# A delta-rule attention and two expert layers on one core: units of three chunks of two sequences, wider scan steps, no filler products in the first unit

## The chip, the cores and the metric

The kernel runs on one core of a Trainium2 chip. The metric is the device time of one execution in microseconds (us); lower is better. The engines named below are TensorE (PE in the rows; its weight loads are PEld), VectorE (DVE), ScalarE (ACT), GpSimd (POOL) and SyncE (SP, which here only issues DMAs).

## What is computed

All data are fp32. The first part is a recurrence along each of 4 x 8 sequences of 768 positions with heads of 48; it is computed in chunks of 64 positions. The second part is a gated dense layer on 3072 tokens of 384 values with 1536 hidden columns. The third sends each token with a positive skip score to one of 8 experts.

```python
# attention: for every batch and head, t = 0 .. 767
y[t] = q[t] @ state
v_old = state.T @ kn[t]                     # kn: k divided by its norm
state += beta[t] * outer(kn[t], v[t] - v_old)
# dense layer: x is y, laid out as 3072 tokens x 384
x = (sigmoid(x @ w_gate) * (x @ w_val)) @ w_out
# experts: rows with x @ w_skip > 0 go to e = argmax(x @ w_gate2)
out = x;  out[row] = x[row] + softmax_weight * (relu(x[row] @ w1[e]) @ w2[e])
```

## The kernel before

The work is cut into Q = 8 units of CT = 384 tokens. A unit of the kernel before is JU = 6 chunks of 64 positions of one batch entry, all 8 heads; two units in a row make a sequence. For each unit TensorE makes the scores of keys and queries (stage `gram`, L682), VectorE masks them (`pt`, L468, and `mask`, L475 to L482), turns them to lanes (L485) and solves the triangular system of every chunk in 30 dependent steps of two instructions (`solve`, L489 and L491). `from_lanes` (L493 to L496) turns the result back; `off` (L698, L712) and `wu` (L728, L731) are products that need it. Then comes the scan over the chunks, in which the state `st` passes from chunk to chunk: `read` (L746) multiplies the state, VectorE subtracts (L516), `write` (L763 and L771) multiplies again, VectorE adds to the state (L521) and ScalarE copies the outputs out (L619), and the next `read` waits for both. `x_turn` (L805 to L810) transposes the unit's outputs for the dense layer, whose pieces are `gate` (L824), `val` (L833) and `out` (L842), three products of 384 or 393 columns each; 12 gates, 12 vals and 12 outs make a unit's dense work.

Every engine runs its own instructions in order, and all of them walk through one list of stages that `program_order` writes. In that list the attention of unit q+1 lies between the dense pieces of unit q, so only unit 0's attention has nothing beside it. `dense(n)` appends pieces, `behind(n)` appends stages that only VectorE has (`lengths`, `mask`, `turn_in`, `solve`), each with a weight. A VectorE stage that stands ahead of another in the list also runs ahead of it, whatever TensorE does. In unit 0 the kernel before puts products that nobody reads (stage `warm`, L790: 128x256 by the identity) between the stages: 20 behind the `router` products (L782), 22 more from `off` to the last `write`, 42 in all.

A small product uses a part of the array (64x64 or 32x64), a dense one all of it. In TensorE's rows of the trace every fp32 product stands as two records, so x6 is three products. The experts' part (L993 to L1108) is not touched by the change.

## Time and profile before

| | us |
|---|---|
| median of 3 runs (lowest to highest) | 1058.85 (1058.5 to 1059.47) |
| the profiled execution | 1058.32 |
| its span in the profile | 1056.5 |
| TensorE busy | 990.5 (94%) |
| VectorE busy | 455.4 (43%) |
| ScalarE busy | 168.4 (16%) |
| GpSimd busy | 109.1 (10%) |

The span is the profiled part of one execution; 1.8 us of its time lie around it. Busy is the time in which an engine has an instruction in work. The first dense piece starts 88.47 us into the span, the last one ends about 834 us in, and the experts follow. TensorE is busy nearly all the time between those two points; ahead of the first it has long idle stretches.

### The profile page before, as it was taken

What the parts mean: (1) busy time and instruction counts of PE and PEld (TensorE: products, weight loads), DVE (VectorE), ACT (ScalarE), POOL (GpSimd) and SP (SyncE); (2) the same over time, 40 slices, a digit from 0 to 9 for tenths busy, and PEclk for the clock granted to TensorE, in tenths of its full rate; (3) what the DMA queues carried; (4) which work ended last, traced back from release to release, by engine and by line L of the source; (5) the groups of instructions that cost most, each with busy time, mean ns of one, the idle gap of its engine ahead of it and who ended that gap; (6) DMA issues with size and microseconds to landing.
All of it is one profiled execution on the core that took longest, in us unless ns stands there. A gap on an engine that the chain in (4) does not pass through costs nothing. (4 is left out here: it accounts for less than half of the span.)

```text
span 1056.5 us, 23056 instructions
## 1 busy us (share of the span) xinstructions
PE 990.5 (94%) x10065; PEld 661.8 (63%) x10065; DVE 455.4 (43%) x1130; ACT 168.4 (16%) x370; POOL 109.1 (10%) x137
## 2 busy tenths in 40 slices
PE   4899999999999999999999999999999539999997
PEld 3776655665665566556656655655555337878785
DVE  5958586385358427624843583112011111111121
ACT  2022211210221022112102210211110011111110
POOL 3010100101010110011010101000001112222221
PEclk9599999999999999999999999999999869999999
DMA  9502003000300210030003000000730104444410
GB/s 349 226 3 106 2 2 136 18 1 17 136 2 1 88 66 1 2 135 18 1 16 137 2 1 20 29 1 1 281 124 1 45 18 155 156 152 152 143 35 27
DMA packets 28859, 74.03 MB, mean 70 GB/s; under 512 B 3912, under 2 KB 19960, under 8 KB 27744
## 3 DMA queue, kind: packets, MB, share of 16 engines
q1 hardware_dynamic: 18672, 56.74, 14.6%
q10 hardware_dynamic: 6912, 9.55, 2.5%
q0 software_dynamic: 3184, 6.39, 2.0%
q8 instruction: 74, 1.21, 0.5%
q14 instruction: 17, 0.14, 0.0%
HBM read 60.62 MB, written 13.00 MB: 70 GB/s over the span
## 5 line engine op out<-in xcount | busy, mean ns | idle before, releaser
L842 PE MATMUL ps<-wo,prod 128*128 128x393 f32 x576 | 205.3, 503 | 3.6 <-DVE prod L535 3.2
L824 PE MATMUL ps<-xT,wg 128*128 128x384 f32 x576 | 205.9, 494 | 0.7 <-ACT xT L626 0.7
L833 PE MATMUL ps<-xT,wv 128*128 128x384 f32 x576 | 206.2, 494 | 0.0
L842 PEld LDWEIGHTS ps<-wo,prod 128*128 128x128 f32 x576 | 104.7, 189 | 74.6 <-DVE prod L535 6.5
L824 PEld LDWEIGHTS ps<-xT,wg 128*128 128x128 f32 x576 | 105.9, 190 | 68.7 <-issue 1.8
L833 PEld LDWEIGHTS ps<-xT,wv 128*128 128x128 f32 x576 | 105.6, 190 | 67.2 <-issue 1.0
L535 DVE TENSOR_TENSOR prod<-sig,ps 128x384 f32<-128x384 f32 x96 | 53.2, 554 | 213.5 <-PE ps L833 212.0
L1094 PEld LDWEIGHTS ps_h<-xgT,arena 128*128 128x128 f32 x816 | 95.0, 194 | 5.2 <-ACT xgT L1051 1.0
L1094 PE MATMUL ps_h<-xgT,arena 128*128 128x128 f32 x816 | 95.3, 277 | 0.6 <-ACT xgT L1051 0.6
L1106 PE MATMUL ps_y<-arena,hT 128*128 128x384 f32 x272 | 90.5, 486 | 0.0
L631 ACT ACTIVATE sig<-ps 128x384 f32<-128x384 f32 x96 | 47.1, 490 | 272.6 <-PE ps L824 272.6
L491 DVE TENSOR_TENSOR arena<-arena 128x30 f32<-128x30 f32 (+14 forms) x240 | 79.7, 332 | 8.2
L489 DVE TENSOR_TENSOR arena<-arena 128x30 f32<-128x30 f32 (+14 forms) x240 | 79.3, 330 | 6.6
L377 POOL DMA_INDIRECT lists<-token,slot x24 | 23.7, 986 | 481.9 <-DVE slot L568 477.1
L1106 PEld LDWEIGHTS ps_y<-arena,hT 128*128 128x128 f32 x272 | 50.4, 190 | 31.5
L349 POOL TENSOR_TENSOR length<-sq,half 128x24 f32<-128x24 f32 x8 | 33.4, 4181 | 296.7 <-DVE sq L452 296.7
L682 PE MATMUL ps<-arena 48*64 48x128 f32 x768 | 29.1, 308 | 17.9 <-DMA arena<-in_kq 9.0
L1041 DVE SCALAR_TENSOR_TENSOR yv<-ps_y,gate,xres 128x384 f32<-128x384 f32 x17 | 10.5, 618 | 81.8 <-PE ps_y L1106 81.8
L1030 DVE TENSOR_SCALAR hT<-ps_h 128x256 f32<-128x256 f32 x34 | 14.4, 425 | 65.7 <-PE ps_h L1094 65.7
L682 PEld LDWEIGHTS ps<-arena 48*64 48x64 f32 x768 | 25.7, 155 | 22.1 <-issue 18.5
L746 PEld LDWEIGHTS ps<-st,arena 48*64 48x64 f32 x1408 | 24.5, 134 | 23.2 <-issue 21.7
L728 PEld LDWEIGHTS ps<-tt,arena 64*64 64x64 f32 x768 | 33.5, 133 | 8.3 <-issue 4.9
(152 smaller groups left out, 835.3 us busy)
## 6 DMA issues: line engine op xcount, KB each, us to landing
arena<-in_moe_w SPq DMA_DIRECT2D x16, 1536.0 KB, 10.4
arena<-in_kq SPq DMA_DIRECT2D x8, 1536.0 KB, 7.6
x_scratch<-x ACTq DMA_DIRECT2D x24, 196.5 KB, 3.6
arena<-in_kr SPq DMA_DIRECT2D x8, 576.0 KB, 3.8
vr<-in_v SPq DMA_DIRECT2D x8, 576.0 KB, 10.0
out<-x ACTq DMA_DIRECT2D x24, 192.0 KB, 3.2
prod<-in_turned_moe_w_out SPq DMA_DIRECT2D x1, 2304.0 KB, 19.3
wo<-in_moe_w_out SPq DMA_DIRECT2D x1, 2304.0 KB, 25.0
```

Of the source, the lines that this page charges most:

```text
L349: nc.gpsimd.tensor_tensor(length[:], sq[:], half[:].to_broadcast([P, NS]), ALU.pow).then_inc(root_ready, 1)
L489: link(nc.vector.tensor_tensor(tv, xl[:, u + 1:H2, u:u + 1].to_broadcast([P, rows, u]), xl[:, u:u + 1, 0:u].to_broadcast([P, rows, u]), AL ...
L491: link(nc.vector.tensor_tensor(xl[:, u + 1:H2, 0:u], xl[:, u + 1:H2, 0:u], tv, ALU.add))
L535: nc.vector.tensor_tensor(prod[:, f, :], sig[:, f % 2, :], ps_m[3 - f % 2][:, 0:CT], ALU.mult)\
L631: nc.scalar.activation(sig[:, f % 2, :], ps_m[f % 2][:, 0:CT], ACT.Sigmoid).then_inc(sig_ready, 1)
L682: last = nc.tensor.matmul(banks[rows(h), c, n * 2 * C:(n + 1) * 2 * C], kq[part, q % 2, j, g, h, 0, :], kq[part, q % 2, j, g, h, :, :].rea ...
L728: nc.tensor.matmul(ps_a[rows(c), 2 + h, k * C:(k + 1) * C], kr[rows(h), q % 2, n * D:n * D + GP], tt[rows(h), n, :], start=True, stop=True)
L824: last = nc.tensor.matmul(ps_m[f % 2][:, 0:CT], wg[:, a, f * P:(f + 1) * P], xT[:, a, :], start=(a == 0), stop=(a == KT - 1))
L833: last = nc.tensor.matmul(ps_m[3 - f % 2][:, 0:CT], wv[:, a, f * P:(f + 1) * P], xT[:, a, :], start=(a == 0), stop=(a == KT - 1))
L842: last = nc.tensor.matmul(ps_m[t][:, 0:XW], prod[:, a, t * P:(t + 1) * P], wo[:, a, :], start=(a == 0), stop=(a == NF - 1))
L1094: last = nc.tensor.matmul(ps_h[f // 2][:, f % 2 * P:(f % 2 + 1) * P], w1[:, ws, a, f * P:(f + 1) * P], xgT[:, a, :], start=(a == 0), stop= ...
L1106: last = nc.tensor.matmul(ps_y[:, 0:DM], hT[:, f, :], w2[:, ws, f, :], start=(f == 0), stop=(f == FT - 1))
```

## The change

It regroups the work. A unit is now JS = 3 chunks of SEQ = 2 sequences (two batch entries), so the tokens of a unit, and the number of products, stay as they were, and four units in a row carry one pair of sequences. The scan has three steps per unit instead of six, each with twice the columns in every instruction: 32 products in a `read`, 16 and 16 in a `write`. The `warm` products are gone. In the list of stages: a dense piece now stands between `wu` and `gram`; VectorE's stages are paid out behind every dense piece in every region, at 0.8 per piece; the gap between scan steps is worked out from what dense work is left. In unit 0 the loads are cut and reordered (`load_first`), ScalarE copies the raw scores to SBUF (`raw`), VectorE's `pt` for units 0 and 1 moves behind the solve and behind the scan, and the first `mask` instruction no longer needs the scores. The output's rows are put back in order on the host. The diff, cut to its core:

```diff
-JU = 6
+JS = 3
+SEQ = 2
+JU = JS * SEQ
...
-    def dense(n):
-        owed[0] += n
-        while pieces and (owed[0] >= 0.5 or pieces[0][0] in light):
-            owed[0] -= pieces[0][0] not in light
-            order.append(pieces.pop(0))
     def behind(n):
         owed[1] += n
@@ -67,46 +64,47 @@
             event, w = later.pop(0)
             owed[1] -= w
             order.append(event)
+        owed[1] = min(owed[1], 0.0)
+    def dense(n):
+        owed[0] += n
+        while pieces and (owed[0] >= 0.5 or pieces[0][0] in light):
+            heavy = pieces[0][0] not in light
+            order.append(pieces.pop(0))
+            if heavy:
+                owed[0] -= 1
+                behind(0.8)
...
+        for j in range(JS):
+            s = q * JS + j
+            if s % (QS * JS):
+                steps.append(("read", s, j))
+            steps.append(("write", s, j))
...
-    order += [("norm", 0, 0), ("lengths", 0, 0), ("gram", 0, 0), ("gram", 0, 1), ("pt", 0, 0), ("gram", 0, 2), ("pt", 0, 1),
-              ("pt", 0, 2)] + [event for event, _ in prepare(0)[1:5]]
-    order += [("gram", 1, i) for i in range(3)] + [("router", 0, 0), ("warm", 0, 20)] + [event for event, _ in prepare(0)[5:]]
-    order += [("from_lanes", 0, 0), ("router_copy", 0, 0), ("off", 0, 0), ("pt", 1, 0), ("pt", 1, 1), ("warm", 1, 4),
-              ("off", 0, 1), ("norm", 1, 0), ("warm", 1, 3), ("wu", 0, 0), ("pt", 1, 2), ("warm", 1, 2), ("wu", 0, 1),
-              ("warm", 1, 2)]
+    order += [("norm", 0, 0)] + [("gram", 0, i) for i in range(3)] + [event for event, _ in prepare(0)[0:5]]
+    order += [("router", 0, 0)] + [("gram", 1, i) for i in range(3)]
+    order += [event for event, _ in prepare(0)[5:]]
+    order += [("from_lanes", 0, 0), ("router_copy", 0, 0), ("off", 0, 0), ("off", 0, 1)]
+    order += [("pt", 0, i) for i in range(3)] + [("wu", 0, 0), ("norm", 1, 0), ("wu", 0, 1)]
     later = prepare(1)
     for step in scan(0):
         order.append(step)
-        if step != scan(0)[-1]:
-            order.append(("warm", 1, 1))
-        behind(0.4)
-        owed[1] = 0.0
-    order += [("x_turn", 0, a) for a in range(KT)]
+        behind(0.5)
+    order += [("x_turn", 0, a) for a in range(KT)] + [("pt", 1, i) for i in range(3)]
...
-            lead = sum(w for _, w in later) / 0.82
             while later:
-                behind(0.82)
-                owed[1] = 0.0
                 dense(1.0)
             follows = q + 1 < Q
-            steps = scan(q)
-            gap = max(0.6, (32.0 - lead - 7.0) / len(steps))
...
             order.append(("wu", q, 1))
+            dense(1.0)
             if follows:
                 order += [("gram", q + 1, 0), ("gram", q + 1, 1), ("pt", q + 1, 0)]
                 dense(1.0)
                 order += [("gram", q + 1, 2), ("pt", q + 1, 1), ("pt", q + 1, 2)]
+                dense(0.7)
                 later = prepare(q + 1)
-            dense(0.7)
+            steps = scan(q)
+            gap = max(0.7, (sum(p[0] not in light for p in pieces) - 4.0) / len(steps))
             for step in steps:
                 order.append(step)
-                behind(0.86 * gap + 0.23)
                 dense(gap)
-                owed[1] = min(owed[1], 0.0)
...
-        first = 2 * (i + 1) if q == 1 else 2 * (i % 2)
+        first = 4 if (q, i) == (0, 2) else 2 * (i % 2)
...
+        load_first(0)
+        load_kr(0)
+        load_first(1)
+        load_first(2)
         sp.dma_start(bt[:], beta_d).then_inc(beta_in, 16)
-        load(0)
-        load(1)
+        sp.dma_start(wr[:, :, 0:1], ws_d.rearrange("(a p o) -> p a o", p=P, o=1), allow_slow_non_contiguous=True).then_inc(router_in, 16)
+        sp.dma_start(wr[:, :, 1:R1], wgt_d.rearrange("(a p) e -> p a e", p=P)).then_inc(router_in, 16)
+        sp.dma_start(wo_t, wo_t_d.rearrange("(a p) f -> p a f", p=P)).then_inc(router_in, 16)
+        load_kq(1)
+        load_kr(1)
         load_v(0)
-        sp.dma_start(wr[:, :, 0:1], ws_d.rearrange("(a p o) -> p a o", p=P, o=1), allow_slow_non_contiguous=True).then_inc(wo_in, 16)
-        sp.dma_start(wr[:, :, 1:R1], wgt_d.rearrange("(a p) e -> p a e", p=P)).then_inc(wo_in, 16)
-        sp.dma_start(wo_t, wo_t_d.rearrange("(a p) f -> p a f", p=P)).then_inc(wo_in, 16)
+        load_v(1)
         sp.dma_start(wo[:, :, 0:DM], wo_d.rearrange("(a p) f -> p a f", p=P)).then_inc(wo_in, 16)
-        load_v(1)
         sp.dma_start(wg[:], wg_d.rearrange("(a p) f -> p a f", p=P)).then_inc(w_in, 16)
...
-                dve.wait_ge(graw_copied, 3 * q + i + 1)
-                pair = gram_banks(q, i).rearrange("p c (j g a t) -> p c j g a t", j=2, g=G2, a=2)
-                own_pt = pt[:, q % 2].rearrange("p (c j g) t -> p c j g t", c=CG, g=G2)
+                own_pt = pt[:, q % 2].rearrange("p (c j g) t -> p c j g t", c=CG, g=G2)[:, :, 2 * i:2 * i + 2]
+                if q < 2:
+                    dve.wait_ge(raw_copied, 3 * q + i + 1)
+                    scores = own_pt
+                else:
+                    dve.wait_ge(graw_copied, 3 * q + i + 1)
+                    scores = gram_banks(q, i).rearrange("p c (j g a t) -> p c j g a t", j=2, g=G2, a=2)[:, :, :, :, 1, :]
                 nc.vector.tensor_tensor(
-                    own_pt[:, :, 2 * i:2 * i + 2], pair[:, :, :, :, 1, :],
-                    tri[:].unsqueeze(1).unsqueeze(1).to_broadcast([P, CG, 2, G2, C]), ALU.mult).then_inc(pt_ready, 1)
+                    own_pt, scores, tri[:].unsqueeze(1).unsqueeze(1).to_broadcast([P, CG, 2, G2, C]), ALU.mult)\
+                    .then_inc(pt_ready, 1)
...
                 diag = dg[:, 0:NS, :]
+                factors = dn[:, 0:NS, :]
                 if i == 0:
+                    if q:
+                        dve.wait_ge(y1_done, q)
+                    nc.vector.scalar_tensor_tensor(
+                        out=factors, in0=tri32[:].unsqueeze(1).to_broadcast([P, NS, H2]), scalar=-1.0,
+                        in1=bp[:, 0:NS].unsqueeze(2).to_broadcast([P, NS, H2]), op0=ALU.mult, op1=ALU.mult)
+                elif i == 1:
                     dve.wait_ge(upper_ready, q + 1)
                     link(nc.vector.scalar_tensor_tensor(out=diag, in0=graw[:, q % 2, :, H2:C], scalar=lower[:, 0:1], in1=diag,
                                                         op0=ALU.mult, op1=ALU.add))
-                elif i == 1:
-                    link(nc.vector.scalar_tensor_tensor(out=diag, in0=diag, scalar=-1.0,
-                                                        in1=bp[:, 0:NS].unsqueeze(2).to_broadcast([P, NS, H2]),
-                                                        op0=ALU.mult, op1=ALU.mult))
                 else:
-                    link(nc.vector.tensor_tensor(diag, diag, tri32[:].unsqueeze(1).to_broadcast([P, NS, H2]), ALU.mult))
+                    link(nc.vector.tensor_tensor(diag, diag, factors, ALU.mult))
...
+                u = u_of(s // JS, i)
+                nc.vector.tensor_tensor(u, u, ps_a[:, 0:2, 0:W4], ALU.subtract).then_inc(u_ready, 1)
             elif stage == "write" and (q + 1) % SB:
                 s = q
                 dve.wait_ge(s_done, writes(s))
                 if s % SB:
-                    nc.vector.tensor_tensor(st[:], st[:], ps_a[:, 2:4, 0:W2], ALU.add).then_inc(st_ready, 1)
+                    nc.vector.tensor_tensor(st[:], st[:], ps_a[:, 2:4, 0:W4], ALU.add).then_inc(st_ready, 1)
                 else:
-                    nc.vector.tensor_copy(st[:], ps_a[:, 2:4, 0:W2]).then_inc(st_ready, 1)
+                    nc.vector.tensor_copy(st[:], ps_a[:, 2:4, 0:W4]).then_inc(st_ready, 1)
...
+        def raw(q, i):
+            pair = gram_banks(q, i).rearrange("p c (n a t) -> p c n a t", n=2 * G2, a=2)
+            nc.scalar.activation(by_group(pt[:, q % 2], 2 * G2 * i, 2 * G2), pair[:, :, :, 1, :], ACT.Copy)\
+                .then_inc(raw_copied, 1)
...
+                if q == 1:
+                    raw(1, i)
+                elif q == 0 and i == 2:
+                    for third in range(3):
+                        raw(0, third)
...
+                if q == 0:
+                    pe.wait_ge(kq_first[i], 16)
+                elif i == 0:
+                    pe.wait_ge(kq_in[q % 2], 16 * ((q + 1) // 2))
+                if q >= 2 and i < 2:
+                    pe.wait_ge((u_evac, w_evac)[i], 2 * q)
+                elif q >= 2:
                     pe.wait_ge(pt_ready, 3 * q + 1)
+                elif q == 1:
+                    pe.wait_ge(raw_copied, (3, 3, 4)[i])
...
+                    for x in range(SEQ):
+                        for g in range(G2):
+                            for c in range(CG):
+                                part = slice(GP * c, GP * c + D)
+                                for h in range(HH):
+                                    o = x * W2 + g * D
+                                    last = nc.tensor.matmul(
+                                        ps_a[rows(h), c, a * W4 + o:a * W4 + o + D], kq[part, b, SEQ * i + x, g, h, a, :],
+                                        st[part, h, o:o + D], start=(a == 0 and x == 0 and g == 0), stop=(a == 0),
+                                        skip_group_check=True)
...
+                if s < JS and i == 0:
+                    pe.wait_ge(pt_ready, 3)
+                for x in range(SEQ):
                     for g in range(G2):
                         for c in range(CG):
-                            n = CN * c + G2 * i + g
+                            n, o = CN * c + G2 * (SEQ * i + x) + g, W4 + x * W2 + g * D
                             for h in range(HH):
-                                last = nc.tensor.matmul(ps_a[rows(c), 2 + h, g * D:(g + 1) * D],
-                                                        kr[rows(h), b, n * D:n * D + GP], vr[rows(h), b, n * D:(n + 1) * D],
-                                                        start=True, stop=True)
-                    last.then_inc(s_done, 1)
-                for g in range(G2):
-                    for c in range(CG):
-                        n = CN * c + G2 * i + g
-                        for h in range(HH):
-                            last = nc.tensor.matmul(ps_a[rows(h), c, W2 + g * D:W2 + (g + 1) * D], pt[rows(h), b, n, :],
-                                                    vr[rows(h), b, n * D:(n + 1) * D],
-                                                    start=(s % SB == 0 and g == 0), stop=True, skip_group_check=True)
+                                last = nc.tensor.matmul(
+                                    ps_a[rows(h), c, o:o + D], pt[rows(h), b, n, :], vr[rows(h), b, n * D:(n + 1) * D],
+                                    start=(s % SB == 0 and x == 0 and g == 0), stop=True, skip_group_check=True)
...
-            elif stage == "warm":
-                if q:
-                    pe.wait_ge(pt_ready, 5)
-                for _ in range(f):
-                    nc.tensor.matmul(ps_m[0][:, 0:2 * P] if q else ps_a[:, 1, 0:2 * P], ident[:], wo_t[:, 0, 0:2 * P],
-                                     start=True, stop=True)
```

TensorE's rows in the order of the program, first unit, from the `router` products on. Before, with L790 the products that nobody reads:

```order
L782 MATMUL ps<-wr,prod 128x9 x36
L790 MATMUL ps<-prod,ident 128x256 x20
L698 MATMUL ps<-arena 64x32 x48
L790 MATMUL ps<-prod,ident 128x256 x4
L712 MATMUL ps<-dt,y 64x32 x48
L790 MATMUL ps<-prod,ident 128x256 x3
```

The same place now, with L817 the router, L714 `gram`, L729 and L741 `off`:

```order
L714 MATMUL ps<-arena 64x128 x48
L817 MATMUL ps<-wr,prod 128x9 x36
L714 MATMUL ps<-arena 64x128 x48
L729 MATMUL ps<-arena 64x32 x48
L741 MATMUL ps<-dt,y 64x32 x48
```

The router moved ahead of unit 1's `gram`, and nothing stands between the stages.

TensorE's rows in the dense work of unit 0 from unit 2's `gram` on (L682), through the scan of unit 1 (L746 `read`, L763 and L771 `write`), before:

```order
L682 MATMUL ps<-arena 64x128 x16
L824 MATMUL ps<-xT,wg 128x384 x3
L746 MATMUL ps<-st,arena 64x48 x16
L833 MATMUL ps<-xT,wv 128x384 x3
L763 MATMUL ps<-vr,arena 64x48 x8
L771 MATMUL ps<-vr,arena 64x48 x8
L824 MATMUL ps<-xT,wg 128x384 x3
L746 MATMUL ps<-st,arena 64x48 x16
```

And now (L714 `gram`, L776 `read`, L795 and L806 `write`, L852, L861 and L872 the dense pieces):

```order
L861 MATMUL ps<-xT,wv 128x384 x3
L714 MATMUL ps<-arena 64x128 x32
L852 MATMUL ps<-xT,wg 128x384 x3
L714 MATMUL ps<-arena 64x128 x16
L861 MATMUL ps<-xT,wv 128x384 x3
L776 MATMUL ps<-st,arena 64x48 x32
L872 MATMUL ps<-wo,prod 128x393 x3
L795 MATMUL ps<-vr,arena 64x48 x16
L806 MATMUL ps<-vr,arena 64x48 x16
L872 MATMUL ps<-wo,prod 128x393 x6
```

Each run of small products in the scan is twice as long, and there are half as many; the first `gram` run has a dense piece ahead of it. From the first dense piece to the end there were 136 runs of small products between dense ones, and there are 102 now: 39 reads became 20, 42 writes became 21, and 6 `gram` runs that stood right behind a `wu` now stand alone.

VectorE's rows around unit 3's `from_lanes`, before (L516 and L521 the last scan step's, L535 the product of gate and val):

```order
L521 TENSOR_TENSOR st<-st,ps 128x192
L516 TENSOR_TENSOR vr<-vr,ps 128x2x96
L521 TENSOR_TENSOR st<-st,ps 128x192
L493 MEMSET arena 128x32
L494 TENSOR_TENSOR arena<-arena,bl 128x1024
L495 STREAM_TRANSPOSE arena<-arena 128x32x32
L496 STREAM_TRANSPOSE dt<-arena 128x32x32
L535 TENSOR_TENSOR prod<-sig,ps 128x384
```

And now (L509 and L511 the last three solve steps, L515 the transpose that `off` waits for, L555 gate times val):

```order
L555 TENSOR_TENSOR prod<-sig,ps 128x384
L509 TENSOR_TENSOR arena<-arena 128x84
L511 TENSOR_TENSOR arena<-arena 128x3x28
L509 TENSOR_TENSOR arena<-arena 128x58
L511 TENSOR_TENSOR arena<-arena 128x2x29
L509 TENSOR_TENSOR arena<-arena 128x30
L511 TENSOR_TENSOR arena<-arena 128x30
L513 MEMSET arena 128x32
L514 TENSOR_TENSOR arena<-arena,bl 128x1024
L515 STREAM_TRANSPOSE arena<-arena 128x32x32
L516 STREAM_TRANSPOSE dt<-arena 128x32x32
```

The solve of units 1 to 3 now ends among the dense pieces, behind a gate-times-val that VectorE can only do when TensorE has finished that `val`; two pieces later on TensorE's list stands the `off` that needs L515.

## Rows read from the trace of the kernel before

**Rows 1.** TensorE's groups from 100 to 825 us: busy, mean, idle before.

```profile
L842 PE MATMUL ps<-wo,prod 128*128 128x393 f32 x550 | 196.7, 503 | 3.6 <-DVE prod L535 3.2
L682 PE MATMUL ps<-arena 48*64 48x128 f32 x576 | 18.5, 273 | 5.7 <-DVE vr L510 5.7
```

**Rows 2.** Timeline of TensorE in unit 1's dense work: start, us, instructions.

```profile
244.25 0.45 PE L763 MATMUL ps<-vr,arena 64*64 64x48 f32 x16
...
245.10 2.20 PE L833 MATMUL ps<-xT,wv 128*128 128x384 f32 x6
247.13 2.10 PE L824 MATMUL ps<-xT,wg 128*128 128x384 f32 x6
249.07 2.10 PE L833 MATMUL ps<-xT,wv 128*128 128x384 f32 x6
251.10 0.68 PE L746 MATMUL ps<-st,arena 48*64 48x48 f32 x32
```

**Rows 3.** Timeline of TensorE around unit 2's gram.

```profile
127.25 1.98 PE L682 MATMUL ps<-arena 48*64 48x128 f32 x64 [0.94 <-DVE vr L510]
129.16 2.20 PE L833 MATMUL ps<-xT,wv 128*128 128x384 f32 x6
131.29 1.10 PE L682 MATMUL ps<-arena 48*64 48x128 f32 x32
132.32 2.20 PE L824 MATMUL ps<-xT,wg 128*128 128x384 f32 x6
```

**Rows 4.** Timeline of the first unit up to its off.

```profile
8.99 3.69 PE L682 MATMUL ps<-arena 48*64 48x128 f32 x64 [8.99 <-DMA arena<-in_kq]
...
14.95 0.18 DVE L462 TENSOR_TENSOR bp<-bp,sq 128x24 f32<-128x24 f32 x1
...
19.61 1.02 DVE L475 SCALAR_TENSOR_TENSOR arena<-arena,lower 128x768 f32<-128x768 f32 x1 [0.33 <-ACT arena L589]
...
24.68 0.20 DVE L489 TENSOR_TENSOR arena<-arena 128x30 f32<-128x30 f32 x1
...
30.67 15.53 PE L782 MATMUL ps<-wr,prod 128*128 128x9 f32 x72 [7.87 <-DMA wo<-in_moe_w_out]
...
45.13 0.24 DVE L489 TENSOR_TENSOR arena<-arena 128x84 f32<-128x84 f32 x1
...
48.09 2.07 DVE L495 STREAM_TRANSPOSE arena<-arena 128x1024 f32<-128x1024 f32 x1
...
56.69 1.60 PE L698 MATMUL ps<-arena 32*64 32x32 f32 x96
```

**Rows 5.** Timeline of the first unit's scan, up to the first dense piece.

```profile
69.92 0.45 PE L763 MATMUL ps<-vr,arena 64*64 64x48 f32 x16
...
71.41 0.68 PE L746 MATMUL ps<-st,arena 48*64 48x48 f32 x32
72.02 0.70 PE L790 MATMUL ps<-prod,ident 128*128 128x256 f32 x2
...
72.65 0.45 PE L763 MATMUL ps<-vr,arena 64*64 64x48 f32 x16
...
85.85 0.58 PE L805 MATMUL ps<-ident,yo 64*128 64x64 f32 x6 [0.42 <-ACT yo L619]
...
88.47 2.17 PE L824 MATMUL ps<-xT,wg 128*128 128x384 f32 x6 [0.67 <-ACT xT L626]
```

**Rows 6.** Stretches of TensorE: length, busy (records), granted clock, DMA share, GB/s.

```profile
44.00:46.00 2.00, 2.00 (x11) 0.50 0.00 0
...
48.00:49.00 1.00, 1.00 (x4) 0.50 0.00 0
...
50.00:51.00 1.00, 1.00 (x7) 1.00 0.00 0
```

**Rows 7.** Two of TensorE's groups from 0 to 100 us: products nobody reads, and wu.

```profile
L790 PE MATMUL ps<-prod,ident 128*128 128x256 f32 x82 | 23.5, 424 | 0.0
...
L731 PE MATMUL ps<-vr,tt 64*64 64x48 f32 x96 | 4.6, 216 | 0.0
```

142 lines of the change are left out of this document (68 added, 74 removed).

## The prediction

> **What bounds the kernel now.** I read the page first (TensorE busy nine tenths and more in nearly every slice), then TensorE's groups from 100 to 825 us. In that stretch its idle time is 3.6 us ahead of `out`, waiting for VectorE's last gate-times-val, and 5.7 us ahead of `gram`, waiting for the copy behind `wu` [rows 1]. So the middle is bound by what TensorE executes, and a gain there has to come from shorter execution or from those waits. Then the timeline of one unit: the reader is to compare pieces that have a dense neighbour with pieces that have a small run beside them [rows 2, 3]. The first unit is another regime: TensorE waits there for VectorE's solve, and from `off` to the first dense piece two engines alternate [rows 4, 5]. Last, the clock in short stretches [rows 6].
>
> **Part 1: fewer runs of small products.** A dense piece that starts behind a small run or ends ahead of one takes 2.03 us from its start to the next start, one in the middle 1.94 [rows 2]. A run of dense pieces thus pays 0.18 for its two ends. A `gram` run of 32 products (x64) takes 1.91 to the next start, one of 16 takes 1.03 [rows 3]: 0.88 for 16 products, 0.15 fixed. Together 0.33 us per run of small products. The order shows 136 such runs before and 102 now, 34 fewer: 34 x 0.33 = **-11.2 us**. The products themselves are as many as before, so nothing else changes on TensorE here. VectorE and ScalarE get twice the elements in half the instructions; behind a dense piece of 2 us that is covered. Without that cover a step pays it, as in the first unit below.
>
> **Part 2: a dense piece between `wu` and `gram`.** The wait of 0.94 in rows 3 is one of six that make the 5.7 us [rows 1]. The copy that `gram` waits for ends within 1 us of `wu`, and a dense piece of 2 us now stands there: **-5.7 us**. Late next would be `pt`, which has one dense piece to hide behind, as before.
>
> **Part 3: VectorE's solve ends among the dense pieces.** In units 1 to 3 VectorE must do gate-times-val, the last solve steps and `from_lanes`, while TensorE does two or three pieces and then stands at `off`. The last three solve steps, the fill, the multiplication and L495 take from 45.13 to 50.16 = 5.0 us [rows 4]. With 0.66 for gate-times-val (an estimate, from the 1.02 of a 768-element instruction in rows 4, halved, and a hand-over) that is 5.7 in unit 3 against two pieces = 3.9 [rows 2]: a wait of 1.8. Unit 1 has two solve steps left in place of three (0.5 less): 1.3. Unit 2 has five (1.2 more) against three pieces = 5.8: 1.1. Behind the late `off` VectorE also does its scaling and norm before the copy that `wu` waits for, some 0.3 more in each. Sum 5.1, less the 0.3 that unit 1 paid before: **+5 us**. In units 4 to 7 no val stands between the scan and `from_lanes`, VectorE runs ahead, and I expect no wait. If instead it arrives late there too, each unit pays up to the 1.8 of unit 3. What queues behind the wait is all of TensorE's list, so it is paid in full.
>
> **Part 4: the first unit up to `off`.** Before, the first mask instruction starts at 19.61, behind VectorE's `pt` and ScalarE's copies, and the solve at 24.68. Now the three `pt` are gone from there and the masks can follow `lengths`, whose last instruction ends at 15.13 [rows 4]. The scores must be there in time: their load is cut in three and comes first; before, all of it had landed by 8.99 [rows 4]. At the pace of the first row, 16 products take about 1.85 us; six copies and the upper half's copy of some 0.6 to 0.9 each then put ScalarE at about 14.5, before its result is wanted at 16.1. So the solve starts 4.5 us earlier, and L495 ends at 50.16 - 4.5 = 45.7. Before, `off` started only at 56.69, because the router's products (30.67 to 46.0, late for their load) and then 20 useless ones stood ahead of it. Now the router's load comes fourth and its 15.5 us are over by about 31, `gram` of unit 1 by 37. `off` starts at 45.7: **-11.0 us**. The cover for the router is the solve; it has some 9 us to spare.
>
> **Part 5: from `off` to the first dense piece, at which clock.** Before, this took 88.47 - 56.69 = 31.8 us [rows 4, 5], at the full clock (granted 1.00, 2.4 GHz), which came after 3.5 us of useless products (0.50, 1.2 GHz, until 49, 1.00 from 50 [rows 6]); in all they cost TensorE 23.5 us of busy time [rows 7], mostly where it had nothing else. Now nothing keeps the array busy while VectorE solves from 37 to 45.7. What is a half clock worth? The first `gram` ran 32 products in 3.69 us, the same run takes 1.91 later [rows 3, 4], so its products double. And the router's 15.5 us of uninterrupted work left the clock at 0.50 (44 to 46 [rows 6]): being busy was not enough. I double all small products:
> - `off` twice 1.5 and `wu` 4.6 [rows 4, 7] are 7.6 at full clock, 15.2 at half. The rest between 56.69 and 69.92, 5.6, is hand-overs to ScalarE and VectorE and some filler; I keep 4.8. Sum 20.0.
> - The scan: a `read` of 16 takes 0.61 [rows 5], of 32 with one fixed part 1.07; S and Y of 8 take 0.85 [rows 2], of 16 then 1.53. A `read` starts 0.64 after the end of the `write`, a `write` 0.63 after the end of the `read` [rows 5]; with twice the elements I put 0.2 on each. Three steps: 3.06 + 0.83 + 2 x (2.14 + 0.83 + 3.06 + 0.83) = 17.6, against 15.9 before (69.92 to 85.85).
> - `x_turn` 2.6 before [rows 5], 4.6 with its products doubled.
> Together 42.2 in place of 31.8: **+10.4**, and the first dense pieces still run at half pace until the clock comes. It took 3.5 us in rows 6; with 4.4 at half pace, **+2.2**. At full clock the same sum is 12.4 + 10.9 + 2.6 and 1.7 for a `mask` that would then stand ahead of a subtraction: 27.6.
>
> **Sum**, against the profile's own 1058.3 (0.5 below the median): 1058.3 - 11.2 - 5.7 + 5 - 11.0 + 10.4 + 2.2 = **1048.0 us**. So the first unit gives nothing (+1.6), and the middle gives 12.
>
> The Trainium skill speaks for the other clock: "TensorE: Matmul & The Clock Gate", Part 1, has the low clock as the default state and sustained activity as what releases it, and `off`, `wu` and the scan are activity. By it the first unit could be at 2.4 GHz from `wu` on, and the time 1031 to 1040. The same page, section "LDWEIGHTS", gives a load's time by its columns without a factor for the clock; by that the small products would hardly slow, with much the same result. The router's rows at 0.50 are against the first reading; of the second no row here shows these shapes at the half clock.
>
> **Rivals.**
> - **The clock comes early, or the small products don't care (24%).** Everything from 45.7 on takes 27.6: the first dense piece at 73.3 in place of 88.5, 15.2 earlier: 1058.3 - 15.2 - 11.9 = 1031. If it comes at the start of the scan only, the scan, `x_turn` and the first pieces save 6.7 + 2.0 + 2.2 of that: 1037. For it: `wu` is 4.5 us of unbroken work at half pace. Against it: the router's 15.5 us, and a hand-over of 1 us between all these stages.
> - **New waits eat the fewer runs (9%).** A wide step leaves VectorE less room: one dense piece between `read` and `write` in places, with masks or solves in its queue. If each of seven units pays 1.4 us more, 10 us go: 1058.
> - **Slower (7%).** VectorE's queue is late at `off` in all seven units, and more than in unit 3. It is 1.8 there; four more units at that price give 1055. It decides from about 3.3 us per unit on: 7 x 3.3 = 23, less the 5 counted, is 1066. For it: behind every dense piece VectorE now gets 0.8 of weight everywhere. Against it: VectorE is busy 43% of the span in the table.
>
> **How the numbers follow.** The forecast has 60%, its own range 1044 to 1052: 2 us for the first dense pieces, 2 for part 3, 1 for part 1. The range for 8 in 10 reaches down to the clock rival, 1031, and up to 1053. Against 1058.85 plus or minus 2 us, about what this kernel's measurement can tell: faster 60 + 24 and about half of the second rival, 0.89; same 0.04; slower 0.07.
>
> **What would show it.** Right: `off` starts near 45.7; the granted clock is 0.50 from there to a few us into the first gate, at 88; runs of 32 `read` products take 1.07; no wait ahead of `gram`; 1 to 2 us ahead of `off` in units 1 to 3 alone. Wrong: a clock of 1.00 in the scan; small runs that cost more than their products; waits ahead of `read` or `write` in the middle.

## The result, and the profile after

The changed kernel takes 1041.6 us (median of 4 runs, 1040.3 to 1042.0) beside 1058.7 for the kernel before in the same measurement: ratio 0.984, 95% interval 0.982 to 0.986. It is faster by 17 us; the forecast was 10.8. The time lies inside the range of 1031 to 1053, but below the forecast's own 1044 to 1052. Two more measurements, below, give 15.2 and 13.9 us. The profiled execution took 1042.03 us, against 1058.32 before: 16.3 less.

The page of the changed kernel, its engines' busy time, in a span of 1040.3 us:

```profile
PE 970.9 (93%) x9983; PEld 657.7 (63%) x9983; DVE 449.3 (43%) x1086; ACT 167.2 (16%) x352; POOL 109.5 (11%) x137
```

The trace splits the 16.3 us. The first dense piece starts at 81.92 in place of 88.47 [rows 5]: **-6.55**. From there to the end of the last `out`: 734.5 us in place of 745.6: **-11.1**. What follows is the experts' part, not touched: 223.9 in place of 222.5: **+1.4** (its first tile meets the clock at 0.50).

The timeline of the changed kernel: start, duration, engine, line, and in brackets the idle time ahead and what ended it. L499 and L515 on VectorE are the first masked solve input and the transpose that `off` waits for; L729 and L741 `off`, L776 `read`, L795 and L806 the two halves of a `write`, L833 the start of `x_turn`, L852 and L861 dense pieces:

```profile
16.05 1.01 DVE L499 SCALAR_TENSOR_TENSOR arena<-arena,lower 128x768 f32<-128x768 f32 x1
...
43.54 2.00 DVE L515 STREAM_TRANSPOSE arena<-arena 128x1024 f32<-128x1024 f32 x1
45.60 2.79 PE L729 MATMUL ps<-arena 32*64 32x32 f32 x96 [9.69 <-DVE arena L515]
...
65.84 1.96 PE L776 MATMUL ps<-st,arena 48*64 48x48 f32 x64 [0.73 <-ACT yo L650]
68.46 1.10 PE L795 MATMUL ps<-vr,arena 64*64 64x48 f32 x32 [0.67 <-DVE vr L536]
69.35 1.92 PE L806 MATMUL ps<-vr,arena 64*64 64x48 f32 x32
...
78.04 0.90 PE L833 MATMUL ps<-ident,yo 64*128 64x64 f32 x6 [0.58 <-ACT yo L650]
...
81.92 4.18 PE L852 MATMUL ps<-xT,wg 128*128 128x384 f32 x6 [0.67 <-ACT xT L658]
85.89 2.27 PE L861 MATMUL ps<-xT,wv 128*128 128x384 f32 x6
...
292.43 1.60 PE L729 MATMUL ps<-arena 32*64 32x32 f32 x96 [1.72 <-DVE arena L515]
293.95 3.76 PE L852 MATMUL ps<-xT,wg 128*128 128x384 f32 x6
297.65 1.56 PE L741 MATMUL ps<-dt,y 32*64 32x32 f32 x88
...
402.15 0.68 PE L795 MATMUL ps<-vr,arena 64*64 64x48 f32 x32
402.65 1.11 PE L806 MATMUL ps<-vr,arena 64*64 64x48 f32 x32
403.69 2.20 PE L861 MATMUL ps<-xT,wv 128*128 128x384 f32 x6
...
413.57 1.15 PE L776 MATMUL ps<-st,arena 48*64 48x48 f32 x64
```

Read from the top. VectorE's mask starts at 16.05 (forecast 16.1, before 19.61), its transpose ends at 45.54 (45.7), and `off` starts at 45.60 after a wait of 9.69 (before 56.69 [rows 4]). The two `off` runs take 2.79 and 2.78, where the same run took 1.60 at full clock [rows 4]. In the scan a `read` of 32 products (x64) takes 1.96 at 65.84 and 1.15 at 413.57; a `write` 2.81 (68.46 to 71.27) and 1.61 (402.15 to 403.76). The first dense piece, 81.92, needs 3.97 to the next start. The three rows at 292 to 297 us, in unit 3, come up below.

The stretches of TensorE in the first unit: length, busy (records), granted clock, DMA share, GB/s:

```profile
44.00:62.00 18.00, 13.34 (x381) 0.50 0.01 3
62.00:64.00 2.00, 0.95 (x43) 0.92 0.00 0
64.00:66.00 2.00, 1.27 (x52) 0.94 0.00 0
66.00:86.00 20.00, 16.67 (x299) 0.50 0.37 138
86.00:88.00 2.00, 2.00 (x7) 0.94 0.04 16
```

From `off` to the first dense piece the clock is at 0.50 (1.2 GHz), but for some 3.4 us between 62 and 66, behind `wu` (0.92 and 0.94 are means over 2 us). The first dense pieces bring 1.00 (2.4 GHz).

The waits of TensorE from 94 to 812 us, as total, times, longest:

```profile
PE ps L729 <- DVE arena L515: 4.1, 3, 1.7
PE ps L872 <- DVE prod L555: 2.9, 4, 0.7
```

Nothing waits ahead of `gram` any more: its 5.7 us [rows 1] are gone. `off` waits three times, in units 1 to 3: 1.3, 1.1 and 1.7.

### The profile page after: what moved, and what is told of

Same layout as the page of the kernel before. It is cut to its first block and busy times, and to the rows that moved or that the text cites. A ratio compares the mean times of both kernels' runs of the same rounds, so it can differ in the third digit from the quotient of the medians.

```text
span 1040.3 us, 22827 instructions
## 1 busy us (share of the span) xinstructions
PE 970.9 (93%) x9983; PEld 657.7 (63%) x9983; DVE 449.3 (43%) x1086; ACT 167.2 (16%) x352; POOL 109.5 (11%) x137
## 5 line engine op out<-in xcount | busy, mean ns | idle before, releaser
L852 PE MATMUL ps<-xT,wg 128*128 128x384 f32 x576 | 208.5, 499 | 0.7 <-ACT xT L658 0.7
L872 PE MATMUL ps<-wo,prod 128*128 128x393 f32 x576 | 203.4, 501 | 2.9 <-DVE prod L555 2.9
L861 PE MATMUL ps<-xT,wv 128*128 128x384 f32 x576 | 204.7, 492 | 0.0
L555 DVE TENSOR_TENSOR prod<-sig,ps 128x384 f32<-128x384 f32 x96 | 53.2, 554 | 252.3 <-PE ps L861 251.9
L852 PEld LDWEIGHTS ps<-xT,wg 128*128 128x128 f32 x576 | 107.9, 192 | 71.9 <-issue 4.0
L872 PEld LDWEIGHTS ps<-wo,prod 128*128 128x128 f32 x576 | 105.3, 189 | 75.1 <-DVE prod L555 5.3
L861 PEld LDWEIGHTS ps<-xT,wv 128*128 128x128 f32 x576 | 107.2, 190 | 71.0 <-issue 1.8
L511 DVE TENSOR_TENSOR arena<-arena 128x30 f32<-128x30 f32 (+14 forms) x240 | 79.7, 332 | 8.2
L509 DVE TENSOR_TENSOR arena<-arena 128x30 f32<-128x30 f32 (+14 forms) x240 | 79.2, 330 | 6.0
L1136 PEld LDWEIGHTS ps_y<-arena,hT 128*128 128x128 f32 x272 | 50.4, 190 | 31.5
L757 PEld LDWEIGHTS ps<-tt,arena 64*64 64x64 f32 x768 | 36.8, 143 | 10.1 <-issue 5.5
L757 PE MATMUL ps<-tt,arena 64*64 64x64 f32 x768 | 39.1, 246 | 2.2 <-DVE tt L525 1.1
L760 PE MATMUL ps<-vr,tt 64*64 64x48 f32 x768 | 40.6, 226 | 0.0
L760 PEld LDWEIGHTS ps<-vr,tt 64*64 64x64 f32 x768 | 38.5, 145 | 0.0
## 6 DMA issues: line engine op xcount, KB each, us to landing
vr<-in_v SPq DMA_DIRECT2D x8, 576.0 KB, 11.1
```

What stands on the lines that cost most here:

```text
L509: link(nc.vector.tensor_tensor(tv, xl[:, u + 1:H2, u:u + 1].to_broadcast([P, rows, u]), xl[:, u:u + 1, 0:u].to_broadcast([P, rows, u]), AL ...
L511: link(nc.vector.tensor_tensor(xl[:, u + 1:H2, 0:u], xl[:, u + 1:H2, 0:u], tv, ALU.add))
L555: nc.vector.tensor_tensor(prod[:, f, :], sig[:, f % 2, :], ps_m[3 - f % 2][:, 0:CT], ALU.mult)\
L757: nc.tensor.matmul(ps_a[rows(c), 2 + h, k * C:(k + 1) * C], kr[rows(h), q % 2, n * D:n * D + GP], tt[rows(h), n, :], start=True, stop=True)
L760: last = nc.tensor.matmul(ps_a[rows(h), c, k * D:(k + 1) * D], tt[rows(h), n, :], vr[rows(h), q % 2, n * D:(n + 1) * D], start=True, stop= ...
L852: last = nc.tensor.matmul(ps_m[f % 2][:, 0:CT], wg[:, a, f * P:(f + 1) * P], xT[:, a, :], start=(a == 0), stop=(a == KT - 1))
```

## The experiments

Each was measured beside the kernel before on the same chip; the ratio is to that. "Middle" is the stretch from the start of the first dense piece to the end of the last `out`. "By terms" is 745.6 us of before, plus 0.33 per run of small products over 136, plus the waits over before's 9.6 (3.6 + 5.7 + 0.3), plus what the clock cost beyond before (the first piece at half pace 2.0, falls in the middle), plus idle moments within `write` and `read` (last section), counted as what these runs take beyond 1.54 and 1.08 each.

| kernel | time, us | ratio, 95% | first dense piece | small runs | waits | clock | idle moments | by terms | middle |
|---|---|---|---|---|---|---|---|---|---|
| changed | 1041.6 | 0.984 (0.982 to 0.986) | 81.92 | 102 | 7.0 | 3.7 | 0 | 735.5 | 734.5 |
| changed, second time | 1043.7 | 0.986 (0.984 to 0.989) | 81.67 | 102 | 7.0 | 2.0 | 3.6 | 737.4 | 736.8 |
| changed, third time | 1044.6 | 0.987 (0.985 to 0.988) | 83.10 | 102 | 7.0 | 2.0 | 3.9 | 737.7 | 737.2 |
| before, bare | 1066.0 | 1.006 (1.004 to 1.008) | 94.27 | 136 | 9.8 | 2.0 | 0 | 747.9 | 748.0 |
| w2 | 1040.5 | 0.982 (0.980 to 0.985) | 80.56 | 102 | 7.0 | 3.7 | 0 | 735.5 | 734.3 |
| w1 | 1034.7 | 0.977 (0.974 to 0.979) | 76.95 | 102 | 7.0 | 3.5 | 0 | 735.3 | 734.1 |
| f3 | 1038.6 | 0.980 (0.977 to 0.982) | 81.75 | 102 | 4.6 | 3.7 | 0 | 733.1 | 731.7 |
| g0 | 1056.2 | 0.996 (0.995 to 0.998) | 81.81 | 95 | 16.6 | 5.1 | 4.4 | 748.6 | 749.3 |
| g0, second time | 1054.9 | 0.996 (0.995 to 0.998) | 80.95 | 95 | 16.5 | 5.0 | 4.8 | 748.8 | 749.4 |
| g0_fill | 1048.7 | 0.990 (0.987 to 0.993) | 80.86 | 95 | 12.9 | 2.0 | 0 | 741.3 | 741.5 |
| g0_piece | 1040.9 | 0.981 (0.978 to 0.985) | 83.10 | 95 | 10.3 | 1.9 | 0 | 734.7 | 734.9 |
| s1, split writes | 1051.4 | 0.992 (0.990 to 0.995) | 80.97 | 118 | 9.6 | 8.4 | 0 | 748.1 | 746.5 |
| best1 | 1029.7 | 0.972 (0.970 to 0.974) | 71.60 | 102 | 2.7 | 1.7 | 5.2 | 734.4 | 732.9 |

(g0_fill has 3.9 us of fillers of its own on top.) The terms meet the middle from 1.6 us above it to 0.7 below.

### The clock in the first unit: before without its fillers, and the changed kernel with some

**Before, bare**: the 42 products nobody reads are left out.

```diff
-    order += [...] + [("router", 0, 0), ("warm", 0, 20)] + [...]
+    order += [...] + [("router", 0, 0)] + [...]
-              ("off", 0, 1), ("norm", 1, 0), ("warm", 1, 3), ("wu", 0, 0), ("pt", 1, 2), ("warm", 1, 2), ("wu", 0, 1),
-              ("warm", 1, 2)]
+              ("off", 0, 1), ("norm", 1, 0), ("wu", 0, 0), ("pt", 1, 2), ("wu", 0, 1)]
...
-        if step != scan(0)[-1]:
-            order.append(("warm", 1, 1))
```

> The kernel before without its 42 products without use and without anything else changed. Clock theory: off starts near 52.2 in place of 56.7, but the six-step scan and what is ahead of it run at 0.50, some 11 us more, and the first dense pieces 2 us more; time 1066 to 1069. Rival (the fillers were worth nothing, they only delayed off): 4 us faster than before, 1054 to 1056.

Measured 1066.0. Its timeline (L695 `off`, L743 `read` of 16, L760 first half of a `write`):

```profile
52.05 2.79 PE L695 MATMUL ps<-arena 32*64 32x32 f32 x96 [6.26 <-DVE wo L525]
...
72.05 1.11 PE L743 MATMUL ps<-st,arena 48*64 48x48 f32 x32 [0.57 <-ACT yo L616]
...
94.27 2.26 PE L821 MATMUL ps<-xT,wg 128*128 128x384 f32 x3 [0.67 <-ACT xT L623]
```

`off` starts 4.6 earlier than before and costs 2.79 again; the granted clock is 0.50 from 44 to 94, and from `off` to the first dense piece it takes 42.2 in place of 31.8. So the fillers of before were worth 7 us net, and small useful products with hand-overs of 0.5 to 1 us between them did not bring the clock in 42 us. A `read` of 16 takes 1.11 against 0.68 [rows 5], a factor of 1.63 and not 2.

**w2**: the changed kernel with 15 fillers (128x256) behind unit 1's `gram`, where TensorE only waits for the solve.

```diff
     order += [("router", 0, 0)] + [("gram", 1, i) for i in range(3)]
+    order.append(("warm", 0, 15))
...
+            elif stage == "warm":
+                for _ in range(f):
+                    nc.tensor.matmul(ps_m[0][:, 0:2 * P], ident[:], wo_t[:, 0, 0:2 * P], start=True, stop=True)
```

> The changed kernel with the 15 products behind unit 1's gram alone, none in the hand-overs. If useful work holds a clock once granted: the clock stays 1.00 to the first dense piece, as with all fillers, about 1031 us. If useful work alone cannot hold it (it came at 62 and was gone at 66 in the changed kernel's profile): it falls to 0.50 somewhere between 46 and 60, first dense piece at 76 to 80, time 1035 to 1040.

Measured 1040.5. Stretches of TensorE in w2, columns as above:

```profile
40.00:46.00 6.00, 4.54 (x48) 1.00 0.11 45
46.00:48.00 2.00, 1.17 (x80) 0.78 0.03 8
48.00:60.00 12.00, 9.77 (x266) 0.50 0.01 3
...
62.00:64.00 2.00, 1.61 (x64) 1.00 0.04 8
```

The fillers bring 1.00, and the first `off` takes 1.60; then, with `off`, `wu` and their hand-overs as only work, the clock falls at 46 to 48, comes for some 3 us behind `wu`, and falls again. So here the useful work brings it for some 3 us and does not keep it. The first dense piece, at 80.56, and the time are both half a us beyond what was expected.

**w1**: the same 15, and one to two fillers in every hand-over.

```diff
-("off", 0, 0), ("off", 0, 1)]
+("off", 0, 0), ("warm", 0, 2), ("off", 0, 1), ("warm", 0, 2)]
-[("wu", 0, 0), ("norm", 1, 0), ("wu", 0, 1)]
+[("wu", 0, 0), ("norm", 1, 0), ("warm", 0, 2), ("wu", 0, 1), ("warm", 0, 2)]
     for step in scan(0):
         order.append(step)
+        if step != scan(0)[-1]:
+            order.append(("warm", 0, 1))
```

> The changed kernel with 15 products without use (128x256) behind unit 1's gram and 1 or 2 in each hand-over from off to the last write of unit 0. Clock theory (from off to the first dense piece small products run at whatever clock is granted, and that is what my first-unit sum missed or hit): off still starts near 45.6, the clock is 1.00 from about 41 on, the first dense piece starts near 73.5 in place of 81.9 and runs at full pace; time about 1031 us. Rival (the stretch is set by hand-overs between engines, the clock gives little, and fillers get in the way): first dense piece at 80 to 82, time 1040 to 1042.

Measured 1034.7. Timeline of w1 (L825 fillers, L732 `off`, L798 the second `write`):

```profile
36.33 6.74 PE L825 MATMUL ps<-prod,ident 128*128 128x256 f32 x30
45.59 2.18 PE L732 MATMUL ps<-arena 32*64 32x32 f32 x96 [2.52 <-DVE arena L518]
...
67.96 0.68 PE L798 MATMUL ps<-vr,arena 64*64 64x48 f32 x32 [1.68 <-DVE vr L539]
...
76.95 3.87 PE L858 MATMUL ps<-xT,wg 128*128 128x384 f32 x6 [0.67 <-ACT xT L661]
```

The fillers end at 43.07, TensorE waits 2.52, and the clock falls within `off` (2.18 for the first, 2.79 for the second); it is back at about 56.5, and the scan runs at full pace. The first dense piece comes 5 us earlier than in the changed kernel, but again at half pace: 3.87, with a granted clock of 0.72 as the mean from 76 to 82. So w1 lies between its two expectations: the fillers reached neither `off` nor the first dense piece without a hole. At 67.96 stands the wait that the prediction's full-clock sum had as 1.7 for a `mask` ahead of a subtraction: 1.68.

### Part 3's wait: one dense piece more ahead of off (f3)

First VectorE in unit 3 of the changed kernel, where `off` waits until 292.43:

```profile
286.97 0.55 DVE L555 TENSOR_TENSOR prod<-sig,ps 128x384 f32<-128x384 f32 x1 [0.37 <-PE ps L861]
...
290.40 1.97 DVE L515 STREAM_TRANSPOSE arena<-arena 128x1024 f32<-128x1024 f32 x1
```

Gate-times-val waits for TensorE's `val`, and from its start to the end of L515 it is 5.4 us, where the prediction had 5.7.

```diff
             order.append(("from_lanes", q, 0))
-            dense(2.0)
+            dense(3.0 if q < 4 else 2.0)
```

> The changed kernel with one more dense piece between from_lanes and off for units 1 to 3. If the three waits of 4.1 us in all ahead of off are paid in full: they go, and the time is 1037 to 1038. Rival (VectorE is late with its whole queue there, the wait moves on to wu or to the scan): 1040 to 1042, with a new wait ahead of wu.

Measured 1038.6. The three waits ahead of `off` (4.1 us) are gone from units 1 to 3, and one of 2.4 in unit 4 is new; timeline of f3 there:

```profile
380.91 1.60 PE L729 MATMUL ps<-arena 32*64 32x32 f32 x96 [2.44 <-DVE arena L515]
382.44 3.90 PE L852 MATMUL ps<-xT,wg 128*128 128x384 f32 x6
386.26 1.60 PE L741 MATMUL ps<-dt,y 32*64 32x32 f32 x96
```

The row behind `off` is to be looked at: a dense piece that takes 3.82 to the next start in place of 2.13. TensorE waited 2.44, did 1.5 us of `off`, and the clock fell. The changed kernel has the same in unit 3: 1.72 of waiting at 292.43, and 3.70 for L852 at 293.95. So a late `off` can cost twice: the wait, and 1.7 us behind it. In two other executions of the changed kernel (below) the same wait was there and the clock stayed at 1.00.

### Part 2 alone: without the dense piece between wu and gram (g0)

```diff
             order.append(("wu", q, 1))
-            dense(1.0)
             if follows:
```

A unit's 36 dense pieces stay; the one that no longer stands there goes into the gaps of that unit's scan, since `gap` is worked out from what is left.

> The changed kernel without the dense piece between wu and gram. By my parts 1 and 2: the wait ahead of gram comes back six times, 5.7 us, while 7 runs of small products fewer (102 to 95) give back 2.3; sum +3.4 us against the changed kernel. Rival (the wait is not worth its 0.9 each, because VectorE's queue is then less full): no wait ahead of gram, 1 to 2 us faster than the changed kernel.

> The changed kernel again, as the yardstick on the same chip as the runs beside it. Both theories: 1040 to 1042 us.

Measured 1056.2 for g0 and 1043.7 for the changed kernel: the one piece, in this place, is worth 12.5 us and not 3.4. TensorE's waits in g0 from 94 to 812:

```profile
PE ps L713 <- DVE vr L529: 5.7, 6, 0.9
PE ps L728 <- DVE arena L514: 5.4, 3, 2.4
PE ps L871 <- DVE prod L554: 4.5, 6, 0.8
```

`gram` waits 5.7 again (L713), `out` 4.5 in place of 2.9, `off` 5.4 in place of 4.1, a `read` 1.0. Together 16.6 against 7.0: 9.6 us, less 2.3 for seven fewer small runs. The clock took more too; timeline of g0 in unit 3:

```profile
293.42 2.18 PE L728 MATMUL ps<-arena 32*64 32x32 f32 x96 [2.39 <-DVE arena L514]
295.53 4.21 PE L851 MATMUL ps<-xT,wg 128*128 128x384 f32 x6
299.67 2.19 PE L740 MATMUL ps<-dt,y 32*64 32x32 f32 x96
301.79 2.20 PE L860 MATMUL ps<-xT,wv 128*128 128x384 f32 x6
```

After 2.39 of waiting `off` takes 2.11 in place of 1.53, the dense piece 4.14 in place of 2.13, the second `off` 2.12 in place of 1.53: 3.2 us. Idle moments make 0.8 more than in the changed kernel beside it; 1.3 of the 12.5 no term holds. So the piece between `wu` and `gram` does more than cover its own wait: without it the waits for VectorE at `off`, `out` and a `read` grow too.

**g0_fill**: g0 with three fillers ahead of `off` in units 1 to 3. **g0_piece**: g0 with one dense piece more between `from_lanes` and `off` in units 1 to 5.

```diff
 g0_fill, in off:
+                    pe.wait_ge(st_ready, writes(JS * q - 1))
+                    for _ in range(3 if q < 4 else 0):
+                        nc.tensor.matmul(ps_a[:, 3, 0:2 * P], ident[:], wv[:, 0, 0:2 * P], start=True, stop=True)
                 pe.wait_ge(dn_ready, q + 1)
 g0_piece:
-            dense(2.0)
+            dense(3.0 if q < 6 else 2.0)
```

> The kernel g0 (no dense piece between wu and gram) with three products without use (128x256, into a bank that the scan has left) ahead of off in units 1 to 3, where TensorE waits 1.2, 1.8 and 2.4 us for VectorE; the waits for VectorE's result stay. If such a wait costs a second time because the granted clock falls behind it (0.50 from 294 to 301 in g0's profile, 3.2 us longer products): no fall in the middle, 2 to 4 us faster than g0, 1052 to 1054. Rival (the clock's fall is not from the wait): as g0 or slower by the fillers, 1056 to 1058, with the fall still there.

> The kernel g0 with one more dense piece between from_lanes and off in units 1 to 5; the wait ahead of gram stays. If g0 lost its time through VectorE's lateness at off and the clock behind it: the 5.4 us ahead of off and the fall go, 5.7 ahead of gram stay, 1047 to 1049. Rival (VectorE's queue is late as a whole and the wait moves to wu, the scan or out): 1052 to 1056.

Measured 1048.7 and 1040.9, both faster than expected. With the fillers the clock did not fall in the middle, and the wait ahead of `off` is 1.7 us in place of 5.4. With the piece all of it is gone: 5.7 ahead of `gram`, 3.6 ahead of `out` and 1.0 ahead of a `read` are left. Part of what both gained beyond the expectation is no doing of the edits: g0's profile holds 4.4 us of idle moments, theirs none.

g0_piece is not told apart from the changed kernel's first measurement (ratio 0.981 and 0.984, intervals that overlap), whose profile has no idle moments either; the two later ones, with them, are 0.986 and 0.987. It keeps the 5.7 ahead of `gram`, has seven fewer small runs and nothing at `off`.

**g0 and the changed kernel once more**, to see whether some 2.6 us of g0's middle, which no wait and no clock row accounts for, belong to it.

> The kernel without the dense piece between wu and gram, run a second time on another occasion, beside the changed kernel: before minus 2.8 us (1056) if the 2.6 us of its middle that no wait and no clock row accounts for belong to the order of its instructions; before minus 5 to 6 us (1053) if they and the engine's idle moments inside runs of small products (0.3 to 0.4 us each, named as issue) belong to the occasion, which would then show none of these idle moments in this profile.

> The changed kernel once more: 0.984 of before (1041.6) if the idle moments inside runs of small products stay away, as in its first profile; 0.986 (1043.7) if they come, as in its second.

Measured 1054.9 and 1044.6. Both had idle moments within `write` again, so the two theories are not told apart by the times. The timelines account for most of it: in g0 one `read` has them too.

```profile
254.83 0.90 PE L775 MATMUL ps<-st,arena 48*64 48x48 f32 x44
...
256.69 0.47 PE L775 MATMUL ps<-st,arena 48*64 48x48 f32 x14 [0.39 <-issue]
257.09 2.25 PE L871 MATMUL ps<-wo,prod 128*128 128x393 f32 x6
```

It takes 2.26 to the next start in place of 1.08, and 2.38 the second time. With 3.2 and 3.5 in the `write`s, the idle moments are 4.4 and 4.8 us, more than the 2.4 and 2.8 that the list of waits names. With them g0's middle is 0.7 and 0.6 longer than the terms, no further off than other rows of the table. In g0_fill, the same order with fillers, both the idle moments and the rest are absent.

### Part 1's price: the writes taken apart (s1)

In units 2 to 7 sixteen of the `write`s are cut into their two halves, with a dense piece between: 118 runs in place of 102, the products the same.

```diff
     for step in scan(0):
         order.append(step)
+        if step[0] == "write":
+            order.append(("finish",) + step[1:])
...
-            gap = max(0.7, (sum(p[0] not in light for p in pieces) - 4.0) / len(steps))
+            split = c >= 1
+            gap = max(0.7, (sum(p[0] not in light for p in pieces) - 4.0 - 3.0 * split) / len(steps))
             for step in steps:
                 order.append(step)
+                if step[0] == "write":
+                    if split and (step[1] + 1) % (QS * JS):
+                        dense(1.0)
+                    order.append(("finish",) + step[1:])
                 dense(gap)
...
                     last.then_inc(s_done, 1)
+            elif stage == "finish":
+                s, b = q, q // JS % 2
```

> The changed kernel with a dense piece between the two halves of 16 writes (S and Y) in units 2 to 7: the same products in 118 runs in place of 102. If a run of small products costs 0.33 us whatever is in it: +5.3 us against the changed kernel, with TensorE never idle for it. Rival (the fixed price per run is an artefact of how records end, and the middle got faster through waits and a shorter scan): within 1 us of the changed kernel.

Measured 1051.4, 7.7 above the changed kernel beside it. Timeline of s1, one split `write` (L802 and L815) with its dense neighbours:

```profile
411.57 0.68 PE L802 MATMUL ps<-vr,arena 64*64 64x48 f32 x32
412.18 2.20 PE L861 MATMUL ps<-xT,wg 128*128 128x384 f32 x6
414.32 1.14 PE L815 MATMUL ps<-vr,arena 64*64 64x48 f32 x32
415.38 2.20 PE L870 MATMUL ps<-xT,wv 128*128 128x384 f32 x6
```

The halves take 0.61 and 1.06, the dense piece between 2.14. Together in the changed kernel they take 1.54 (402.15 to 403.69), and a dense piece among its like 1.94. So one more run costs 0.61 + 1.06 + 2.14 - 1.54 - 1.94 = **0.33 us**, the price of Part 1. Sixteen are 5.3. The rest is not the runs': `off` waits 7.4 in place of 4.1, and the clock falls in units 3 and 4. The whole middle gives much the same price: it is 12.0 longer than in the changed kernel's first profile (746.5 against 734.5), 2.6 of it waits and 4.7 clock, which leaves 4.8 for the sixteen, 0.30 each. Within 1 us of the changed kernel, the rival of the expectation, it is not.

### A version that beats both (best1)

w1 with 18 fillers, others behind each scan step and behind `x_turn`, the `lengths` and `mask` of unit 1 behind the first subtraction, and the longer stretch ahead of `off`.

```diff
+    order.append(("warm", 0, 18))
-("off", 0, 0), ("off", 0, 1)]
+("off", 0, 0), ("warm", 0, 2), ("off", 0, 1), ("warm", 0, 3)]
...
         order.append(step)
-        behind(0.5)
+        order.append(("warm", 0, 1))
+        behind(0.0 if step == scan(0)[0] else 1.0 if step == scan(0)[1] else 0.5)
-    order += [("x_turn", 0, a) for a in range(KT)] + ...
+    order += [("x_turn", 0, a) for a in range(KT)] + [("warm", 1, 2)] + ...
-            dense(2.0)
+            dense(3.0 if q < 6 else 2.0)
```

> The changed kernel with products without use in all of the first unit's gaps (18 behind unit 1's gram, 1 to 3 in every hand-over, 2 behind x_turn), lengths and the first mask of unit 1 behind the first subtraction, and one more dense piece between from_lanes and off in units 1 to 5. Clock theory: 1.00 from before off through the first dense pieces, first dense piece at 72 to 74 at full pace (-10 us against the changed kernel), waits ahead of off gone (-4): 1027 to 1029 us. Rival (the clock falls between off and wu anyway): first dense piece at 76 to 80, 1031 to 1035 us.

Measured 1029.7 (1028.6 to 1030.0), ratio 0.972: 29 us below before, and 14 below the changed kernel beside it. Timeline of best1 (L731 `off`, L857 and L866 dense pieces):

```profile
45.65 1.60 PE L731 MATMUL ps<-arena 32*64 32x32 f32 x96 [0.71 <-DVE arena L517]
...
71.60 2.10 PE L857 MATMUL ps<-xT,wg 128*128 128x384 f32 x6
73.53 0.81 PE L866 MATMUL ps<-xT,wv 128*128 128x384 f32 x2
```

`off` takes 1.60, the first dense piece 1.93 to the next start: full pace from 45.65 on, granted clock 1.00 from 44 to 74. From `off` to the first dense piece it is 25.95 us; the prediction's sum at full clock without its 1.7 was 25.9. The time is just above the 1027 to 1029 expected; its profile holds 5.2 us of idle moments and a fall of the clock in the middle (last section), which the expectation had not.

## Why the prediction was right, and where it was off

**Part 1 (-11.2).** Right. 102 runs, and for each 0.33 us by the rows of s1, 0.30 by its whole middle. A `read` of 32 takes 1.08 to the next start (forecast 1.07), a `write` 1.54 (1.53). The Trainium skill, "TensorEngine Tiling (Array Packing)", section "Key Properties", says that a change of the tiling mode drains the engine; it names no price. The 0.33 of a visit of small products among dense ones is in keeping with that, but no run here tells a drain from another fixed cost.

**Part 2 (-5.7).** The wait ahead of `gram` is gone, as forecast. As a term it is right only with the rest of the change in place: taking the piece out gave back 12.5 us, and with another piece ahead of `off` (g0_piece) it is worth nothing measurable. All the waits that come and go in these runs are for VectorE; what a dense piece is worth on TensorE's list depends on where it stands ahead of them.

**Part 3 (+5).** The waits of 1.3, 1.1 and 1.7 stand where forecast (1.3, 1.1, 1.8), in these three units alone, and f3 shows that a piece more removes them there, at the price of one of 2.4 in unit 4. In unit 3 VectorE's rows bear the mechanism out, with 5.4 us for 5.7. The 0.3 more at `wu` did not come: 3.8 in place of 5. Not priced was what the wait does to the clock: 1.7 us behind the one in unit 3, in the first profile.

**Part 4 (-11.0).** Right: `off` at 45.60, behind VectorE's L515 and not behind TensorE's own list.

**Part 5 (+10.4, +2.2): the term that was mis-sized.** The mechanism is right: the fillers gone, the clock is at 0.50. But the stretch is 36.3 us in place of 42.2. "I double all small products" is the step that failed. The rows that it rested on were `gram`, of 128 columns, 3.69 against 1.91. Taken alike, from record to record, they are 3.69 against 1.98, 1.86 times; and the profile shows a granted clock of 1.00 for that first `gram`, so that it ran at half was a reading of its length alone. The products of 32 to 64 columns that make this stretch take 2.79 against 1.60 (`off`), 1.96 against 1.15 (`read`), 2.81 against 1.61 (`write`), and `wu` 8.2 against the 4.65 of best1: 1.70 to 1.76 times. `off` and `wu` make 13.8 in place of 15.2 and their four hand-overs 4.1 in place of 4.8: 17.9 for 20.0. The scan is 14.6 for 17.6: 1.45 because its first `write` met the clock that came for some 3.4 us, 0.5 for the other two, 0.4 for the `read`s, 0.8 because a hand-over is 0.58 to 0.74 and not 0.83. `x_turn` is 3.9 for 4.6. The first dense pieces cost +2.0 (forecast +2.2).

The sum of it: 5.9 less in Part 5, 1.4 less in the middle (waits 1.9 less than forecast, `out`'s 0.7 among them, 0.2 at the first pieces and 1.0 that no term holds, against 1.7 for the clock's fall), and 1.4 more in the experts' part, which I had left alone. 1048.0 - 5.9 - 1.4 + 1.4 is the profile's 1042.0 within 0.1. That the last two cancel is luck, and that the clock's fall of 1.7 is nearly made up by waits that did not come is too. The forecast's own range, 1044 to 1052, was missed by Part 5, to which it gave only the 2 us of the first dense pieces; the wider range holds because it was drawn down to a rival that did not happen.

**The rivals.** That the clock comes early: no, but half of its second name, that the small products care less, is what moved the time. The Trainium skill, "TensorE: Matmul & The Clock Gate", Part 1, says that sustained activity releases the throttle; here `off` and `wu`, busy 13.3 of the 18 us from 44 to 62, had it released for some 3.4 us, the scan did not keep it, and in the kernel before without fillers such work ran 42 us at 0.50, while dense fillers brought 1.00. So the rule decides nothing until it is known what counts as activity. Its section "LDWEIGHTS" gives a load no factor for the clock; the 1.70 to 1.76 of these rows lie between that and my 2, nearer to mine. New waits in the middle and a VectorE late in all seven units did not come in the changed kernel; g0 shows how near they were: one dense piece fewer, and 12.5 us of the gain go.

## What to carry to other kernels

When two engines pass work to each other in turn and the clock has dropped, don't double the whole stretch: hand-overs stay, and short products grow by less than long ones, so take the factor from a row of the same shape. Dense products that nobody reads pay for themselves where the engine only waits and the waits are short (7 us in the kernel before, some 12 from the changed kernel to best1: 10 by which the first dense piece comes earlier, 2 by its pace), but they must reach without a hole from there through the hand-overs to the first dense work. And a dense piece that covers another engine's queue can be worth more, or less, than the wait that it stands in front of (12.5 us and about nothing, for a wait of 5.7): look at where the slow engine is next asked for.
